# A fused attention and mixer block on one core: when SyncE asks for each pair's transfers

## What is computed

```python
# attention, per head: 8 global keys and a causal window of 96
keep = is_global | is_local
scores = scale * q @ k.T - slope * dist          # masked where not keep
a = softmax(scores)
x = (a @ v)                                      # laid out as batch, 768, 512
# mixing over the positions, then a feed-forward block
u = x + (x.T @ U @ V).T                          # rank 32
u = u + relu(u @ w_ch1) @ w_ch2                  # 512 -> 2048 -> 512
# second block, with each position mixed with the one before it
xk = mu_k * u + (1 - mu_k) * u_prev
xr = mu_r * u + (1 - mu_r) * u_prev
out = sigmoid(xr @ w_r) * (relu(xk @ w_k) ** 2 @ w_v)
```

## Time and profile before

| | |
|---|---|
| median of 3 executions | 537.68 us |
| the three executions | 537.55, 537.68, 540.39 us |
| the profiled execution | 540.11 us, span 538.3 us |
| PE busy | 519.9 us, 97% of the span |
| POOL, DVE, ACT busy | 251.1, 188.5, 137.5 us |
| mean granted clock of TensorE | 0.993 of full speed |
| moved by DMA | 33.85 MB, mean 63 GB/s |
| chain that ended last | PE 96%, issue 2%, DVE 1%, DMA 1% |

### The profile page before, as it was taken

One profiled execution on the slowest core, in us unless ns is written; L12 is line 12 of the kernel. 1 busy time (PEld: TensorE's weight loads), 2 busy tenths in 40 slices (PEclk: granted clock), 3 DMA queues, 4 the chain that ended last, 5 costly groups with the idle time before them and its releaser, 6 DMA issues.

```text
span 538.3 us, 11016 instructions
## 1 busy us (share of the span) xinstructions
PE 519.9 (97%) x4304; PEld 490.6 (91%) x4304; DVE 188.5 (35%) x527; ACT 137.5 (26%) x384; POOL 251.1 (47%) x263
## 2 busy tenths in 40 slices
PE   4888999999999999999999999999999999999997
PEld 3777888899999999999999999999998998998996
DVE  5755777321223222322213222121442342342223
ACT  4755777211111111111111111112321321321321
POOL 3244455556004500049900469920896797798000
PEclk9988999999999999999999999999999999999999
DMA  6744666204000400004420000000001001001001
GB/s 212 279 168 152 241 227 209 83 0 153 4 0 0 157 0 0 0 0 157 156 78 0 0 0 0 1 0 1 0 1 58 0 0 59 1 0 58 0 0 58
DMA packets 15345, 33.85 MB, mean 63 GB/s; under 512 B 1488, under 2 KB 1872, under 8 KB 15312
## 3 DMA queue, kind: packets, MB, share of 16 engines
q1 hardware_dynamic: 14736, 32.57, 17.2%
q10 hardware_dynamic: 576, 0.84, 0.5%
HBM read 30.25 MB, written 3.15 MB: 62 GB/s over the span
## 4 chain that ended last, share of the span: by engine, by line
PE 96%; issue 2%; DVE 1%; DMA 1%; POOL 0%; ACTq 0%; DVEq 0%; POOLq 0%
PE psum L550 25%; PE psum L562 25%; PE psum L606 12%; PE psum L615 12%; PE psum L630 6%; PE psum L410 4%; PE psum L422 4%; PE psum L444 3%; PE psum L436 1%; PE psum L452 1%; PE psum L461 1%; DMA k_in<-in_k 1%; PE psum L458 1%; PE psum L459 1%; DVE probs L844 0%
## 5 line engine op out<-in xcount | busy, mean ns | idle before, releaser
L959 DVE SCALAR_TENSOR_TENSOR HL<-psum,HH 128x384 fp32r<-128x384 f32 x64 | 35.7, 558 | 174.6 <-ACT HH L743 174.6
L743 ACT ACTIVATE HH<-psum 128x384 fp32r<-128x384 f32 x64 | 31.5, 492 | 233.2 <-PE psum L550 233.2
L550 PE MATMUL psum<-UH,w1h 128*128 (+1 forms) x256 | 86.3, 337 | 0.0
L562 PE MATMUL psum<-HH,w2h 128*128 128x384 f32 x256 | 86.1, 336 | 0.0
L562 PE MATMUL psum<-HL,w2h 128*128 128x384 f32 x256 | 86.1, 336 | 0.0
L550 PE MATMUL psum<-UH,w1l 128*128 (+1 forms) x256 | 86.0, 336 | 0.0
L550 PE MATMUL psum<-UL,w1h 128*128 (+1 forms) x256 | 85.9, 335 | 0.0
L562 PE MATMUL psum<-HH,w2l 128*128 128x384 f32 x256 | 85.8, 335 | 0.0
L1082 POOL TENSOR_SCALAR w1h<-raw 128x2048 fp32r<-128x2048 f32 x4 | 7.7, 1919 | 126.2 <-PE psum L562 126.2
L562 PEld LDWEIGHTS psum<-HH,w2h 128*128 128x128 f32 x256 | 48.1, 188 | 0.2 <-issue 0.2
L562 PEld LDWEIGHTS psum<-HL,w2h 128*128 128x128 f32 x256 | 48.1, 188 | 0.0
(11 more groups left out here) (118 smaller groups left out, 949.0 us busy)
## 6 DMA issues: line engine op xcount, KB each, us to landing
v_in<-in_v SPq DMA_DIRECT2D x16, 384.0 KB, 6.1
raw<-in_moe_w_ch SPq DMA_DIRECT2D x6, 1024.0 KB, 5.2
v_rest<-in_v_rest SPq DMA_DIRECT2D x8, 384.0 KB, 5.0
out<-result SPq DMA_DIRECT2D x12, 256.0 KB, 2.1
k_in<-in_k SPq DMA_DIRECT2D x7, 432.0 KB, 3.9
q_in<-in_q SPq DMA_DIRECT2D x7, 384.0 KB, 3.0
raw<-in_moe_w_ch SPq DMA_DIRECT2D x8, 256.0 KB, 7.4
raw<-in_moe_w_v SPq DMA_DIRECT2D x2, 1024.0 KB, 5.1
```

The lines of the kernel that those rows point to most:

```text
L550: mm = pe.matmul(bank[4 + f % 2][:, 0:BLK], w[:, kt, f * P:(f + 1) * P], x[:, kt, ds(blk * BLK, BLK)], start=kt == 0 and n == 0, stop=kt = ...
L562: mm = pe.matmul(bank[d][:, 0:BLK], w[:, f, d * P:(d + 1) * P], x[:, f % 2, :], start=f == 0 and n == 0, stop=f == FQ - 1 and n == 2)
L743: act.activation(HH[:, f % 2, :], bank[4 + f % 2][:, 0:BLK], ACT.Relu).then_inc(hid_high, 1)
L959: dve.scalar_tensor_tensor(out=HL[:, f % 2, :], in0=bank[4 + f % 2][:, 0:BLK], scalar=0.0, in1=HH[:, f % 2, :].bitcast(F32), op0=ALU.max, ...
```

## The change

SP's order alone is edited. load_v is cut into load_rest (the rest values) and load_main (one group of the main values). A pair's loop now runs from p = 0 and asks in three parts: queries and keys of pair p+1 as before; when the scores of 3p+1 units are made, the rest values and the first group of main values of pair p; when those of 3p+2 units are made, the second group and weight quarter p-1 (for p = 0 the mixing factors and mu). The waits that guard the buffers stay.

```diff
-            def load_v(p):
+            def load_rest(p):
                 sp.dma_start(v_rest[:, p % 2, :, :, :, :], vr[p]).then_inc(v_landed[p % 2], 16)
-                for j in range(GROUPS):
-                    sp.dma_start(v_in[:, p % 2, j, :, :, :], vm[p][:, j, :, :, :]).then_inc(v_landed[p % 2], 16)
+
+            def load_main(p, j):
+                sp.dma_start(v_in[:, p % 2, j, :, :, :], vm[p][:, j, :, :, :]).then_inc(v_landed[p % 2], 16)
...
             sp.wait_ge(qk_in[0], 32)
-            load_qk(1)
-            load_v(0)
-            sp.dma_start(U[:, :, :], mix_u).then_inc(uv_in, 16)
-            sp.dma_start(v_rows[:, :], mix_v).then_inc(uv_in, 16)
-            load_v(1)
-            sp.dma_start(mu[:, :, :], mus).then_inc(mu_in, 16)
-            for p in range(1, PAIRS):
+            for p in range(PAIRS):
                 if p + 1 < PAIRS:
-                    sp.wait_ge(qk_done, UNITS * p)
-                    sp.wait_ge(qk_in[(p + 1) % 2], 32 * ((p + 1) // 2))
+                    if p > 0:
+                        sp.wait_ge(qk_done, UNITS * p)
+                        sp.wait_ge(qk_in[(p + 1) % 2], 32 * ((p + 1) // 2))
                     load_qk(p + 1)
+                sp.wait_ge(qk_done, UNITS * p + 1)
                 if p > 1:
                     sp.wait_ge(pv_done, UNITS * (p - 1))
                     sp.wait_ge(v_landed[p % 2], 48 * (p // 2))
-                    load_v(p)
-                load_piece(p - 1)
+                load_rest(p)
+                load_main(p, 0)
+                sp.wait_ge(qk_done, UNITS * p + 2)
+                load_main(p, 1)
+                if p == 0:
+                    sp.dma_start(U[:, :, :], mix_u).then_inc(uv_in, 16)
+                    sp.dma_start(v_rows[:, :], mix_v).then_inc(uv_in, 16)
+                    sp.dma_start(mu[:, :, :], mus).then_inc(mu_in, 16)
+                else:
+                    load_piece(p - 1)
             load_piece(PIECES - 1)
```

## The result

The changed kernel takes 531.37 us in the median of 4 executions (531.21 to 534.58), the kernel before 537.62 (4 executions, 536.49 to 540.39): a ratio of 0.9892, 95% interval 0.9848 to 0.9937. Run a second time, beside 13 executions of the kernel before, it took 531.13 for 538.17, 0.9896 (0.9857 to 0.9935). The forecast was 529.6 us with a range of 528.3 to 534.5. Before and after, the medians differ by 6.3 us. The profiled execution took 531.21 us at a span of 529.4; both are 8.9 us under the profiled execution before, which was itself 2.4 us over its median.

The account below looks back on a forecast made before the run. PE, busy for 97% of the span, was taken as the bound, losing time to late instruction refills. The profiled 540.11 us less 10.77 gained plus 0.3 cost gave 529.6 us, range 528.3 to 534.5.

Parts of the forecast that it names:

- The cause of the stops: PE's "issue" stops in the attention: instruction refills wait behind transfers issued ahead of them; some 6.8 us of stops.
- The gain: Attention's score groups, up to 63.10 us: all 10.77 us lost to stops, half clock and restarting is won.
- the undisturbed time: Attention: a pair of three steps without stops takes 9.99 us on PE.
- (a): Each pair's last value part, asked for later: lands in 4 to 4.5 us, needed after 5.86, no wait.
- The rival that ended slower: Weighted sum waits for late values: 2.9 us for 7 pairs if landing takes 8.8, 550 us; chance 0.07.
- (c): End of attention: a 1,024 KB weight chunk queues behind last values and quarters, delaying a refill: 0 to 1.9 us, taken 0.3.
- POOL's end: End of attention: POOL's last weight-quarter split moves with PE, staying 0.63 us before the first hidden matmul.
- What is left is a run without stops: Whole execution: if the median execution lost 2.4 us less, the end is the same, 529.6 us.
- The rules against it: Instruction refills: skill's 2,048-instruction store, or DMA engines taking turns between queues, would make the change win 0.

Follow-up runs that it names:

- added matmuls: Kernel before with 48 quick small matmuls ahead of the first score group, DMAs untouched: 537.44 us, 0.9979.
- two bursts: Kernel before with, from pair 2 on, queries and keys as before, then all values and the weight quarter one step later: 531.41 us, 0.9875.
- the loop: Kernel before with its start kept (pairs 0 and 1 asked for at once) and the three parts from pair 2 on: 531.64 us, 0.9865.
- the late burst: Kernel before with its whole burst of six issues (2,224 KB) one step later, behind the pair's first score group: 532.63 us, 0.9904.
- the three orders with added matmuls: Three parts, two bursts and the late burst, each with 48 quick matmuls ahead of the first score group: 533.24, 531.93 and 532.48 us.
- the small-values run: Kernel before, same six issues a pair, but most of the values left out from pair 2 on (1,264 KB a burst): 532.38 us, 0.9871.
- the start alone: Changed kernel's order for pairs 0 and 1 only, one burst a pair from pair 2 on as in the kernel before: 538.27 us, 1.0014.

## Why the prediction was right, point by point

- **The cause of the stops** (refills of PE's instructions behind transfers) holds. Fewer bytes at the same instants end the stops, added instructions move them, and the refill's packet now comes 0.1 to 2.8 us after it is due instead of up to 5.2 (behind the start; in it one still waited 4.5). "Issued ahead of it" was too narrow: the longest stop with added matmuls belongs to a refill due 0.3 us before the burst.
- **The gain** between the profiled executions was put at 10.77 us; 8.86 came. Between the medians 8.1 was forecast and 6.3 came. The step that was mis-sized is "I take all of it, because a refill asked for in the worst place has one part ahead of it (at most 2.6 us)". That is true from pair 3 on, and only from there do pairs take the undisturbed time. In the start the parts of pairs 0 to 2 follow one another without a pause, since pairs 0 and 1, the factors and pair 2's queries are all needed within 25 us; the refill due at 12.2 waited 4.5 us, and those of 19.1, 24.3 and 29.5 some 2.5 each. It leaves 1.9 us: a stop of 0.8, one of 0.3, a score group of 1.2 us for 0.9 at 23.4, and steps slowed around them. The 0.64 us by which PE started sooner was lost again, as the score group at 11.50 took 1.69 us where it had taken 0.96.
- **Values** (a): 4 to 4.5 us to landing was forecast. v_in's transfers took 3.1 at least, 4.6 in the median, 5.8 at most, under the 5.86 us of cover, and PE never waited for them. The rival that ended slower needed 7.1.
- **The chunk** (c), put at 0.3 us, cost nothing: the refill due at 81.8 had its packet 2.0 us later, and PE went on without a stop.
- **POOL's end** kept its distance: the last split of a quarter ends at 90.09, the first hidden matmul is at 90.72, 0.63 us as before.
- **What is left is a run without stops** was nearly right for three of the four executions (531.2 to 531.5). The fourth took 534.58 with a mean clock of 0.993, as the profiled one before: the clock can still fall, but no trace shows where it fell there.
- **The rules against it.** The Trainium skill (Runtime: NRT & Kernel Launch, Instruction fetch mechanics) would have PE 2,048 instructions ahead. These runs disagree: a refill whose packet comes 4.5 us after it is due stops PE, and it does so 256 instructions after it is due. The Trainium skill (DMA: Bandwidth & Descriptors, Queues, rings and completion order) has the DMA engines take turns between queues packet by packet. Some 500 packets of queue 1 (1.41 MB) went by while the refill due at 25.04 waited, so it did not get the next turn. That a refill still comes out inside a part in most cases (0.6 MB moved while it waited, after 24.4) doesn't exclude turns altogether.
- **What the prediction did not see** is that the size of the parts is only one way. A burst of 2,224 KB one step later gives 532.6, and two bursts 531.4. The kernel before had its bursts where a refill came with five or six issues ahead of it, and for the first of them PE had only 4.8 us of instructions left.

## What to carry to other kernels

When PE stops inside a group of equal matmuls and the profile calls it "issue", count the instructions between stops, and look for the packet of the instruction queue in the DMA view: a fixed count and a late packet mean a refill behind a burst. Then spread the burst over the steps that have slack, or move it within what its data allow; measure both, since either may do. Refill stops cost twice when the clock falls behind them, and they vary from execution to execution, so compare medians of several.

## What had not been expected of the hardware

- The same kernel, before the change, took 534.0 to 543.5 us over the executions of all groups; the changed one 530.7 to 535.5. Of its executions in the groups of the loop and of the late burst, the seven without a fall of the clock (mean clock 1.0) took 534.0 to 536.4 and those at 0.990 to 0.994 mostly 538 to 542: by these the falls explain some half of the gain, the stops alone the other. In the group of the three orders with added matmuls three executions at 1.0 took 536.2 to 539.6, so the share is not settled.
- 192 small float32 matmuls one after the other (64x64 of 64 columns, all on one quarter of the array) took 20.64 us, 107 ns each. The 32 of a score group, spread over the four quarters, took 1.72 us just behind them (at 25.85), 54 ns each, and 0.91 us, 28 ns each, from 34.76 on. So the fair neighbour is 54 ns; the number of columns differs too, and how much the quarters give is not shown.
- A stop of 1.71 us was followed by a fall of the clock and one of 1.91 was not; in the small-values run one of 2.7 us was. One of 2.18 us was followed by a fall in the kernel with the start alone and was not in the one with the loop alone, so the length of a stop does not decide it by itself.
